# Strassen's form for an output product, with folded weights and a fifth tile ahead

## The reference

```
h = x @ w_in                                  # 1152 x 512 @ 512 x 2048
layer 1: g = (a0 + a1 h + a2 h^2 + a3 h^3) / (1 + |b0||h| + |b1|h^2 + 1e-6)
layer 2: g = h * tanh(softplus(h))
y = g @ w_out                                 # 1152 x 2048 @ 2048 x 512
```

## Time and profile before

| | us |
|---|---|
| median of 3 runs | 471.25 (469.7 to 475.39) |
| the profiled execution | 470.82, span 469.0 |
| TensorE busy | 454.7 (97%) |
| VectorE busy | 388.4 (83%) |
| ScalarE busy | 306.2 (65%) |
| GpSimd busy | 210.0 (45%) |

### The profile page before, as it was taken

The page is one execution under the profiler, slowest core; times in us unless marked ns, Lnnn a source line. Parts: engine busy times, 40 slices in busy tenths (PEclk is TensorE's granted clock), DMA queues, the critical chain, the costliest instruction groups (busy, mean ns, idle before and its releaser), DMA issues.

```text
span 469.0 us, 10932 instructions
## 1 busy us (share of the span) xinstructions
PE 454.7 (97%) x4312; PEld 332.8 (71%) x4312; DVE 388.4 (83%) x658; ACT 306.2 (65%) x565; POOL 210.0 (45%) x228
## 2 busy tenths in 40 slices
PE   6997999999999999999999999999999999999997
PEld 5776878887888889899999975444445555557663
DVE  5777799999769787676879988889999888878894
ACT  4568798988657784778777777654745555554543
POOL 3878549874625313111227547258652222212122
PEclk9999899999999999999999999999999999999999
DMA  7998647323123000020011411112100200000101
GB/s 134 168 283 247 145 95 195 93 66 74 34 63 80 1 3 3 1 91 1 3 46 25 157 46 50 41 46 95 40 1 0 92 0 2 0 1 1 67 3 45
DMA packets 46544, 29.80 MB, mean 64 GB/s; under 512 B 31900, under 2 KB 40092, under 8 KB 46492
## 3 DMA queue, kind: packets, MB, share of 16 engines
q1 hardware_dynamic: 44972, 28.57, 23.1%
q10 hardware_dynamic: 1520, 0.53, 0.5%
HBM read 26.73 MB, written 2.36 MB: 62 GB/s over the span
## 4 chain that ended last, share of the span: by engine, by line
PE 86%; POOL 6%; DMA 3%; ACT 2%; SPq 1%; issue 1%; DVE 0%; ACTq 0%; POOLq 0%
PE bank L629 38%; PE bank L673 20%; PE bank L653 19%; PE bank L592 3%; DMA work<-in_moe_w_out 2%; POOL w L1103 1%; DMA late<-in_v 1%; PE bank L497 1%; POOL work L1101 1%; POOL g_l L1115 1%; PE bank L515 1%; PE bank L578 1%; POOL late L1103 1%; PE bank L533 1%; POOL late L1067 1%
## 5 line engine op out<-in xcount | busy, mean ns | idle before, releaser
L1115 POOL TENSOR_TENSOR g_l<-work,g_h 128x512 f16<-128x512 f32 (+2 forms) x81 | 88.4, 1092 | 224.2 <-ACT g_h L804 203.3
L629 PE MATMUL bank<-x_h,w 128*128 128x256 f16 (+1 forms) x640 | 102.3, 264 | 1.7 <-DVE x_l L941 1.6
L653 PE MATMUL bank<-g_h,w 128*128 128x256 f16 (+1 forms) x640 | 101.3, 262 | 0.6 <-POOL g_l L1115 0.6
L629 PE MATMUL bank<-x_h,late 128*128 128x512 f16 (+2 forms) x384 | 96.9, 326 | 0.0
L794 ACT ACTIVATE bank<-work,coef 128x512 f32<-128x512 f32 (+2 forms) x81 | 52.4, 647 | 66.9 <-DVE work L971 64.0
L673 PE MATMUL bank<-late,g_h 128*128 128x512 f16 x288 | 92.0, 379 | 0.0
L629 PE MATMUL bank<-x_l,w 128*128 128x256 f16 (+1 forms) x320 | 84.4, 264 | 0.0
L653 PE MATMUL bank<-g_l,w 128*128 128x256 f16 (+1 forms) x320 | 83.8, 262 | 0.0
L653 PEld LDWEIGHTS bank<-g_h,w 128*128 128x128 f16 x640 | 60.9, 98 | 8.6 <-issue 2.8
L629 PEld LDWEIGHTS bank<-x_h,w 128*128 128x128 f16 x640 | 61.3, 98 | 7.5 <-issue 1.9
L629 PE MATMUL bank<-x_l,late 128*128 128x512 f16 (+2 forms) x192 | 62.6, 326 | 0.0
(11 more groups left out here) (103 smaller groups left out, 776.9 us busy)
## 6 DMA issues: line engine op xcount, KB each, us to landing
raw<-in_moe_w_in SPq DMA_DIRECT2D x10, 512.0 KB, 4.5
raw<-in_moe_w_out SPq DMA_DIRECT2D x10, 512.0 KB, 4.0
late<-in_k SPq DMA_DIRECT2D x16, 144.0 KB, 3.9
late<-in_v SPq DMA_DIRECT2D x8, 288.0 KB
late<-in_moe_w_out SPq DMA_DIRECT2D x4, 512.0 KB, 4.3
late<-in_moe_w_in SPq DMA_DIRECT2D x4, 512.0 KB, 4.1
out<-w SPq DMA_DIRECT2D x8, 256.0 KB, 2.5
late<-in_v SPq DMA_DIRECT2D x15, 97.5 KB
```

The lines of the kernel that those rows point to most:

```text
L629: last = pe.matmul(ps, w_in(l, wp)[:, kk, at], x[:, kk, t0:t0 + n], start=(kk == 0 and wp == 0 and x is x_h), stop=(kk == KD - 1 and wp == 1))
L653: last = pe.matmul(ps, w_out(0, wp)[:, f, 128 * d:128 * (d + 1)], g[q % 4][:, i * n:(i + 1) * n], start=False, stop=(f == FT - 1 and d % 2 ...
L1115: pool.tensor_tensor(g_l[q % 4][:, 0:w], num[q % 4][:, 0:w], g_h[q % 4][:, 0:w], ALU.subtract).then_inc(g_rest, 1)
```

## The change

The output product of layer 2 takes Strassen's form (Winograd's variant) on blocks of 2 x 2: two slices f by two rows of 128 tokens of g, and two slices f by two halves of 256 columns of w_out. Instead of eight products of such pieces there are seven, of sums of pieces. The blocks of layer 2 are now 256 tokens four times, each tile two slices, and a last one of 128 tokens, four slices a tile, without Strassen's form; 37 tiles.

- The weights' sums: for each of the 8 odd units of layer 2 GpSimd makes four sums of 256 columns in two steps (`fold`, `fold_rest`); ScalarE makes the head of 1,024 + 768 elements, VectorE the rest of as many. All heads and rests of layer 2 have new ticks, between 100 and 141, and VectorE makes all folded rests and half of the plain ones.
- The sums of g: after g is made, GpSimd adds up four sums (256, 128 and 128 columns), ScalarE makes the head of 384 plain and of 512 summed columns, GpSimd their rests.
- VectorE's numerator and denominator of layer 2 are ordered anew: ScalarE puts e + 2 in PSUM (`factor`), so that VectorE's operations but the first have one operand there.
- y of layer 2: seven results in four banks; ScalarE copies the first, VectorE combines them in seven additions. A bank is open for the next block when `y2_left` says so.
- LAG is 5: five hidden products go ahead of the first output product. STAGES for the attention are as before.

```diff
-    LAG = 4
+    LAG = 5
     BLOCKS1 = [(0, 256), (256, 256), (512, 256), (768, 192), (960, 192)]
-    BLOCKS2 = [(0, 512), (512, 384), (896, 256)]
+    BLOCKS2 = [(0, 256), (256, 256), (512, 256), (768, 256), (1024, 128)]
...
-    tiles += [(1, b, t0, n, min(2, WIDE // n), f) for b, (t0, n) in enumerate(BLOCKS2)
-              for f in range(0, FT, min(2, WIDE // n))]
-    tiles[-1:] = [(1, b, t0, n, 1, f) for _, b, t0, n, _, f0 in tiles[-1:] for f in (f0, f0 + 1)]
+    tiles += [(1, b, t0, n, WIDE // n, f) for b, (t0, n) in enumerate(BLOCKS2) for f in range(0, FT, WIDE // n)]
+    tiles[-1:] = [(1, b, t0, n, 2, f) for _, b, t0, n, _, f0 in tiles[-1:] for f in (f0, f0 + 2)]
...
+    PAIRED = [q for q, (l, _, _, n, _, _) in enumerate(tiles) if l == 1 and n == 256]
+    HW = DM // 2
+    FOLDS = 7
+    PRODUCTS = [(0, 0, 0, 0), (2, 2, 0, 1), (5, 5, 1, 0), (3, 1, 1, 1), (4, 4, 2, 0), (6, 3, 2, 1), (1, 6, 3, 0)]
...
+              ("pool", "fold", (98.9, 103.9, 108.9, 113.9, 118.9, 123.9, 128.9, 133.9)),
+              ("pool", "fold_rest", (100.9, 105.9, 110.9, 115.9, 120.9, 125.9, 130.9, 135.9))]
...
-             (16, 85.4, 103.05, 123.625, 1),
-             (17, 192.562, 96.875, 119.0, 1),
-             (18, 192.975, 102.9, 111.125, 0),
...
-             (31, 234.425, 165.475, 166.875, 1)]
+             (16, 127.14, 100.3, 101.3, 0),
+             (17, 127.145, 103.9, 105.1, 0),
+             (18, 127.147, 104.3, 105.3, 1),
+             (19, 127.15, 108.9, 110.1, 0),
...
+             (31, 127.505, 138.9, 140.1, 0)]
...
+        def folded(j, part):
+            home, at = (w2, 2 * WH + 2 * FOLDS * HW * j) if j < 4 else (w1, 4 * KD * 256 * (j - 4))
+            at += FOLDS * HW * part + (HW if j < 4 and (j > 0 or part == 1) else 0)
+            return home[:, at:at + FOLDS * HW]
...
+        end = late[:, LATE + 2048:LATE + TAIL]
+        g_own = [[sb(f"g_{x}{i}", [128, WIDE], F16) for i in range(4)] for x in "hl"]
+        g_wide = [[end[:, 192 * (4 * x + i):192 * (4 * x + i + 1)].bitcast(F16) for i in range(4)] for x in range(2)]
+        sums = [end[:, 1536 + 512 * i:2048 + 512 * i] for i in range(2)]
...
                 _, b, t0, n, many, f0 = tiles[q]
-                pe.wait_ge(g_rest, q + 1)
-                if b == 0:
-                    wait_rest(pe, FT + f0 // 2 * 2 + 1)
-                for i in range(many):
-                    f = f0 + i
-                    for t in range(n // 128):
-                        row = y2_first[b] + t
-                        if f == 0 and row >= 4:
-                            wait_row(pe, row - 4)
-                        elif f == 0:
-                            pe.wait_ge(y_rest, 2 * len(BLOCKS1) if row >= 2 else 2 * APART + 2)
-                        for wp, g in ((0, g_h), (0, g_l), (1, g_h)):
-                            last = pe.matmul(y2_bank[row % 4][:, :], g[q % 4][:, i * n + 128 * t:i * n + 128 * (t + 1)],
-                                             w_out(1, wp)[:, f, :], start=(f == 0 and wp == 0 and g is g_h),
-                                             stop=(f == FT - 1 and wp == 1))
-                        if q == NT - 1 and row == ROWS - 2:
-                            last.then_inc(row_whole, 1)
+                pe.wait_ge(g_rest, g_parts(q))
+                paired = n == 256
+                for j in range(f0 // 2, (f0 + many) // 2):
+                    if b == 0:
+                        wait_rest(pe, FT + 2 * j + 1)
+                        pe.wait_ge(w_cleared, 1)
+                    own = 256 * (j - f0 // 2)
+                    single = [(own, 0, 0, 0), (own + 128, 2, 0, 1), (own, 4, 1, 0), (own + 128, 3, 1, 0)]
+                    for i, (gi, wi, bank, half) in enumerate(PRODUCTS if paired else single):
+                        first = j == 0 and (i == 0 or (PRODUCTS if paired else single)[i - 1][2] != bank)
+                        if first and b == 0:
+                            pe.wait_ge(y_rest, 2 * len(BLOCKS1) if bank >= 2 else 2 * APART + 2)
+                        elif first:
+                            pe.wait_ge(y2_left, 4 * (b - 1) + bank + 1)
+                        ends = i + 1 == len(PRODUCTS if paired else single) or (PRODUCTS if paired else single)[i + 1][2] != bank
+                        last_one = j == FT // 2 - 1 and ends
+                        for wp, x in ((0, 0), (0, 1), (1, 0)):
+                            g = g_piece(x, q, gi) if paired else g_own[x][q % 4][:, gi:gi + 128]
+                            begin, whole = first and wp == 0 and x == 0, bank < (3 if paired else 1)
+                            if begin and whole:
+                                pe.matmul(y2_bank[bank][:, :], g, beside_zeros(wi), start=True, stop=False)
+                            else:
+                                last = pe.matmul(y2_bank[bank][:, HW * half:HW * (half + 1)], g,
+                                                 folded(j, wp)[:, HW * wi:HW * (wi + 1)], start=begin,
+                                                 stop=last_one and wp == 1)
+                        if last_one and i + 1 < len(PRODUCTS if paired else single):
+                            last.then_inc(y2_done, 1)
...
             def weight_head(u):
...
+                if is_folded(u):
+                    j = u % FT // 2
+                    act.wait_ge(w_folded, 4 * (j + 1))
+                    if j >= 4:
+                        act.wait_ge(h_ready, N1 - FT // 2 + 2 * (j - 4) + 2)
+                    act.activation(folded(j, 0)[:, 0:2 * DM], stage[slot], ACT.Copy, scale=WS)
+                    act.activation(folded(j, 0)[:, 2 * DM:FOLDS * HW], w_sums[j % 2], ACT.Copy, scale=WS).then_inc(w_head, 1)
...
-                    act.activation(d, ps, ACT.Exp, scale=1.0 / HS).then_inc(h_read, 1)
+                    act.wait_ge(den_done, q - 1)
+                    act.activation(ab[q % 2][:, 0:w], ps, ACT.Exp, scale=1.0 / HS).then_inc(h_read, 1)
+            def factor(q):
+                w = width(q)
+                act.wait_ge(g_done, q - 1)
+                act.wait_ge(h_read, q + 1)
+                act.activation(inv_bank[q % 2][:, 0:w], ab[q % 2][:, 0:w], ACT.Identity, bias=two).then_inc(factor_done, 1)
...
+            def head_sums(q):
+                act.wait_ge(g_sums, 3 * (PAIRED.index(q) + 1))
+                act.activation(g_h[q % 4][:, :], sums[q % 2], ACT.Copy).then_inc(g_head, 1)
...
+                    act.wait_ge(y2_done, 3 * b + 1)
+                    act.activation(at, y2_bank[0][:, 0:HW], ACT.Copy, scale=1.0 / YS).then_inc(y2_first_put, 1)
...
             def weight_rest(u):
...
+                if is_folded(u):
+                    j = u % FT // 2
+                    for x, own, left in ((stage[slot_of[u]], slice(0, 2 * DM), 1), (w_sums[j % 2], slice(2 * DM, FOLDS * HW), 0)):
+                        ins = dve.scalar_tensor_tensor(out=folded(j, 1)[:, own], in0=x, scalar=WS, in1=folded(j, 0)[:, own],
+                                                       op0=ALU.mult, op1=ALU.subtract)
+                        ins.then_inc(w_part if left else w_rest[0], 1)
+                    return
...
-                        dve.tensor_scalar(d, d, EXP_20, None, ALU.min).then_inc(clamped, 1)
+                        dve.tensor_scalar(d, ab[q % 2][:, 0:w], EXP_20, None, ALU.min).then_inc(clamped, 1)
...
-                        dve.scalar_tensor_tensor(out=d, in0=d, scalar=2.0, in1=d, op0=ALU.add,
+                        dve.wait_ge(factor_done, q - N1 + 1)
+                        dve.scalar_tensor_tensor(out=d, in0=inv_bank[q % 2][:, 0:w], scalar=EXP_20 + 2.0, in1=d, op0=ALU.min,
                                                  op1=ALU.mult).then_inc(den_done, 1)
                 elif layer == 0:
...
+                c21, c22, c11, c12 = [rows[:, DM * row + HW * i:DM * row + HW * (i + 1)] for i in range(4)]
+                add(c11, p[1], c21).then_inc(y2_left, 1)
+                dve.wait_ge(y2_done, 3 * b + 2)
+                add(c22, p[2], c21).then_inc(y2_sum, 1)
+                dve.wait_ge(y2_sum, 2 * b + 1)
+                add(c21, p[3], c22).then_inc(y2_left, 1)
+                dve.wait_ge(y2_done, 3 * b + 3)
+                add(c12, p[4], c22).then_inc(y2_sum, 1)
+                dve.wait_ge(y2_left, 4 * b + 2)
+                dve.wait_ge(y2_sum, 2 * b + 2)
+                add(c22, p[4], c21).then_inc(y2_last, 1)
+                add(c12, p[5], c12).then_inc(y2_left, 1)
+                dve.wait_ge(y2_last, b + 1)
+                dve.wait_ge(y_added, last_tile[1, b] + 1)
+                add(c21, p[6], c21).then_inc(y2_left, 1)
...
+                b11, b12, b21, b22, t1, t2, t4 = blocks_of(j)
+                pool.tensor_tensor(t1, b12, b11, ALU.subtract).then_inc(w_folded, 1)
+                pool.wait_ge(w_folded, 4 * j + 1)
+                pool.tensor_tensor(t2, b22, t1, ALU.add).then_inc(w_folded, 1)
+            def fold_rest(j):
+                b11, b12, b21, b22, t1, t2, t4 = blocks_of(j)
```

(45 more changed lines are left out.)

152 lines of the change are left out of this document (95 added, 57 removed).

## The result

The changed kernel takes 561.05 us (median of 4 runs, 552.25 to 564.11) against 472.41 before (4 runs, 469.70 to 475.39). The ratio, taken from the undisturbed runs alone (two of the four after), is 1.179, interval 1.171 to 1.187. I had forecast 486.5 and a range of 467 to 499. The direction was right, but the kernel lost 88.6 us where I had 15.7, between five and six times as much. The profiled execution is the one of 552.25 us.

What follows compares the result with a forecast made beforehand. TensorE's streamed columns were taken as the bound, with the chain through ScalarE, VectorE and GpSimd close behind. The sum was 470.8 - 7.5 + 7.0 + 13.2 + 3.0 = 486.5 us, range 467 to 499.

Steps and rivals of the forecast that it cites:

- 1, TensorE's columns: Layer 2's matmuls: output products 8.2 us less, hidden products 0.7 more, net -7.5 us, bound -2.4.
- Rival D: TensorE's matmuls of 128 columns cost what those of 192 do, on top of the forecast: 491.6 us; chance 0.10.
- 2, the fifth tile: Hidden products one output product earlier: waits before hidden(4), hidden(16) and hidden(24), +7.0 us, bounds 2.5 and 9.
- 3, the folding: Layer 2's weight units, ticks 100 to 140: VectorE overdrawn, TensorE waits on h_done, +13.2 us, bounds 6.0 and 20.9.
- 4 and 5, layer 2: Steady tiles of 4.9 us cost 0; leaving y2 at four block borders costs 0.75 each, +3.0 us, bounds 0 and 6.
- A: The extra work is mostly taken in, only the low bounds are paid: 472 us, up to 478; chance 0.17.
- B: The columns decide, the fifth tile takes up VectorE's overdraft: 465.8 us, or 468.8; chance 0.20.
- C: Faster by over 2%, if VectorE's additions in tiles 24 to 40 stay under 13.7 us: 460.2 us; chance 0.08.

Runs made afterwards that it cites:

- e4: The kernel before with five hidden products ahead instead of four (LAG = 5), nothing else: 527.49 us, ratio 1.108.
- e6: The changed kernel, still LAG = 5, with the ticks of ScalarE's, VectorE's and GpSimd's tile work one slot earlier: 513.73 us, ratio 1.085.
- e5: The changed kernel with four hidden products ahead instead of five (LAG = 4), nothing else: 516.27 us, ratio 1.096.
- g3: The changed kernel with four hidden products ahead up to output product 24, then five; folded heads 1.5 and rests 1.2 ticks later: 495.18 us, ratio 1.044.
- g4: g3 with layer 2's units spread, a folded one every 7.5 ticks, a plain one every 5, loads reordered to match: 493.46 us, ratio 1.043.
- g2: The changed kernel with four ahead up to output product 24, then five; GpSimd's sums do 8 columns in place of 256: 497.57 us, ratio 1.051.

## Why the prediction was wrong, point by point

**1, TensorE's columns: right.** TensorE's timeline of the changed kernel, first matmuls of a hidden product of 256 columns, of a Strassen product, of the next hidden one, then of the last block's with 128 columns and the output product behind it:

```profile
380.27 0.27 PE L682 MATMUL bank<-x_h,late 128*128 128x256 f16 x1
...
382.89 0.82 PE L736 MATMUL bank<-late 128*128 128x256 f16 x6
...
385.18 0.27 PE L682 MATMUL bank<-x_h,late 128*128 128x256 f16 x1
...
516.86 0.22 PE L682 MATMUL bank<-x_h,late 128*128 128x128 f16 x1
...
519.54 0.71 PE L736 MATMUL bank<-w,late 128*128 128x256 f16 x5
```

An output product takes 385.18 - 382.89 = 2.29 us, as worked out, and 48 matmuls of 128 columns take 2.68, 56 ns each. Rival D falls, and the trace disagrees with the 81 ns that the Trainium skill ("TensorE: Matmul & The Clock Gate", back-to-back issue gap) gives for this form. Against e4, which is like it in the products ahead, layer 2 is 2.6 us shorter (175.0 to 177.6); -7.5 and +3.0 were forecast. The wait of output product 40, named under points 4 and 5, is 2.0 us of what is missing.

**2, the fifth tile: the step that failed.** I counted three single waits, 7.0 us with an upper bound of 9. They are there, and about as long as forecast: 2.6 before hidden(4), where I had 2.8, and 2.7 and 1.2 on x_l, where I had 2.6 and 1.6. (A third wait on x_l, of 1.3 us before output product 0, stood there before, with 1.6.) But I wrote that "every hidden product now stands one output product earlier" and then asked only what x needs. Each of them also needs h_done of the tile two before. In the plan that is VectorE's part at `pe_tick(m + 1)`, and the hidden product of m + 5 is at `pe_tick(m + 0.5)`; before, h_done stood at `pe_tick(m)`. So in the slots with attention steps the two wait for each other: 23.3 us in 10 waits between output products 0 and 24.

A second wait turned round with it, and I did not count it either. `leave_y` comes LAG iterations behind the last tile of its block, so with LAG = 5 ScalarE and VectorE make it one iteration later. For the first output product of block b, which stands at `pe_tick(8 b)` and needs the bank, VectorE now frees it behind its part at `pe_tick(8 b + 1)` instead of `pe_tick(8 b)`. Output products 8 and 16 stood 6.4 and 2.5 us for it, the 8.9 us of line 1143 above; before, neither waited, and with the other engines shifted (e6) neither waits. Output product 40 has the same kind of wait, 2.0 us, and none with four ahead (e5).

The sum for the stretch: 23.3 on h_done, 8.9 on y, 3.9 on x_l and 0.7 else make up the 36.9 us of idle time; less the 1.4 of before, and with the 12.0 us of longer busy time, they are the 47.5. Up to output product 24 e4 lost 52.4 us in all, with the 2.6 us wait before hidden(4) and the 2.6 us of the product itself. The trace of before had the slack: between h_done and its hidden product it was 0.2 to 0.9 us for the first three tiles and 2 to 7 for most of the next, less than what was taken away, one output product and the attention steps between.

**3, the folding: the mechanism in part, the size wrong.** 13.2 was forecast, with an upper bound of 20.9, and 33.6 measured. Three things were mis-sized or left out. The waits of VectorE for ScalarE's heads, which I took as half of a wait each, 3.6 in all with an upper bound of 7.2, measured 11.0, and in three of the eight units GpSimd's sums stood at their head; moving the work behind h_done (g3) gave back 11.1 us. The folded rests, which I counted with 8 x 2.1 = 17 us, took 23.6: 10.2 for the eight of 1,024 elements and 13.4 for the eight of 768, 1.67 us each instead of the 0.91 in proportion. The estimate in proportion fits where GpSimd is mostly idle beside them (0.95 us, three cases in g4); in the changed kernel GpSimd was at work through seven of the eight. Line 961's successor (L1058) has a mean of 932 ns in this stretch (0.62 alone), about the 0.3 that I had added. And the clock, which I had named among the signs but left out of the sum, is about 10 us: TensorE was busy 11.0 us longer, of which the 48 more but narrower matmuls are 0.8 by the rates of point 1, an estimate. I had VectorE as the full engine; it was at 84%.

**4 and 5, layer 2: nearly right.** Its steady tiles last 4.91 us, all waits hidden. At the block borders TensorE stood for parts of a microsecond each:

```profile
417.68 0.38 PE L734 MATMUL bank<-late 128*128 128x512 f16 x1 [0.23 <-DVE w L1107]
...
419.57 0.39 PE L734 MATMUL bank<-late,g_h 128*128 128x512 f16 x1 [0.21 <-DVE w L1107]
```

That border costs 0.8 us over a steady tile, the next 1.5, the third 0.8; +3.0 for four was about right. Not foreseen was output product 40's wait of 2.0 us for the last y of layer 1.

**The rivals** A, B and C were on the side of less and share the error of point 2; D, on the side of more, fell. None of them said that the added head start could be worth less than nothing.

## What to carry to other kernels

A program order written as ticks holds only for the distance for which it was made: whoever moves one engine's work ahead has to write down, for every wait of the moved instruction, the tick of what it waits for on the other engine, and see that it is still the smaller one; here the formulas of the plan show both waits that turned round (h_done and the leaving of y), though not how long they would be. An engine's spare time per tile bounds what can be added to it only if the additions stand behind what others wait for: the same work cost 11 us less after its heads moved by 1.5 ticks and its rests by 1.2. And a form that saves multiplications has to be charged with what its operands' preparation displaces, as well as with the preparation itself.

## What the runs showed of the hardware that was not expected

The waits' second price: with waits of 2 to 6 us about every 10 us the granted clock was at one half for 51 of 550 us (6 of 469 before), and the same 1905 matmuls took 170.6 us of busy time instead of 158.5. The clock stayed at 1.00 through the stretches of before in which TensorE was at 20.00 of 20. Waiting does not always bring it down: in g3 it stayed at 1.00 from 260 to 280 us with TensorE busy for 15.33 of 20.

GpSimd's work beside a VectorE operation: the folded rest of 768 elements took 0.95 us in three cases of g4, with GpSimd busy beside it for a third of the time or less, 1.21 to 1.36 in the other five with GpSimd busy nearly throughout, and 1.67 in all eight of the changed kernel. That GpSimd's work is the cause is not shown: the one run that cut it (g2, short sums) left other work of GpSimd beside these rests, and they took 1.67 there too.
